# Attention stage of a three-stage kernel: the outputs of a unit in front of the transposes of unit u-2, the first expert matrix loaded two units later, its high parts made in units 8 and 9

## What is computed

```python
# attention: q, k, v are (4, 8, 576, 64)
kv = np.einsum('bhsd,bhse->bhde', k, v)
out = np.einsum('bhsd,bhde->bhse', q, kv)
rms = np.sqrt(np.mean(out * out, axis=-1, keepdims=True) + 1e-06)
x = out / rms * g_norm                       # then heads side by side: x is (2304, 512)
# dense mixture, 4 experts, w1 (512, 1024), w2 (1024, 512)
for e in range(E):
    out += p[:, e:e + 1] * (np.maximum(x @ w1[e], 0.0) @ w2[e])
# then a routed mixture: one of 8 experts for each row
```

## Time and profile before

| | us |
|---|---|
| median of 3 runs | 1134.98 |
| lowest and highest run | 1133.81, 1137.16 |
| the profiled execution, its time | 1131.23 |
| span of that execution (first to last instruction) | 1129.6 |

### The profile page before, as it was taken

One profiled execution on the slowest core, in us unless ns is written; L12 is line 12 of the kernel. 1 busy time (PEld: TensorE's weight loads), 2 busy tenths in 40 slices (PEclk: granted clock), 3 DMA queues, 4 the chain that ended last, 5 costly groups with the idle time before them and its releaser, 6 DMA issues.

```text
span 1129.6 us, 18534 instructions
## 1 busy us (share of the span) xinstructions
PE 1110.4 (98%) x6144; PEld 972.7 (86%) x6145; DVE 728.1 (64%) x1183; ACT 456.2 (40%) x814; POOL 653.3 (58%) x608
## 2 busy tenths in 40 slices
PE   8999999999999999999999999999999999999997
PEld 8888899988998898988998898889977888888885
DVE  4877887888775878888875878888753222222221
ACT  4773454444634444444534444444332222222221
POOL 2586877799868777799868777778331111111101
PEclk9999999999999999999999999999999999999999
DMA  9955778777712358777812258777398259479970
GB/s 242 264 153 185 269 267 288 281 251 273 262 38 75 109 167 304 276 258 271 273 41 75 93 179 303 254 272 266 134 376 315 84 202 393 138 307 383 344 279 15
DMA packets 103073, 252.97 MB, mean 224 GB/s; under 512 B 8318, under 2 KB 48254, under 8 KB 94811
## 3 DMA queue, kind: packets, MB, share of 16 engines
q1 hardware_dynamic: 98080, 237.54, 60.8%
q0 software_dynamic: 4720, 14.46, 3.5%
q10 hardware_dynamic: 203, 0.05, 0.0%
HBM read 173.09 MB, written 79.98 MB: 224 GB/s over the span
## 4 chain that ended last, share of the span: by engine, by line
PE 92%; DVE 3%; ACT 2%; DMA 1%; issue 1%; POOL 0%; SPq 0%; POOLq 0%; DVEq 0%; ACTq 0%
PE ps L1403 29%; PE ps L1405 28%; PE ps L1404 28%; PE ps L1591 2%; PE ps L1361 1%; PE ps L1568 1%; DMA q<-in_q_dram 1%; PE ps L1483 1%; PE ps L1331 1%; DMA row_tile<-dispatched_rows 1%; PE ps L1508 1%; DVE x_rows L1034 0%; DVE attn_rows L955 0%; PE ps L1372 0%; PE ps L1344 0%
## 5 line engine op out<-in xcount | busy, mean ns | idle before, releaser
L1403 PE MATMUL ps<-x_ops_hi,w_hi 128*128 128x384 f32 x672 | 226.4, 337 | 1.9 <-DVE sum L1004 1.9
L1403 PE MATMUL ps<-w_hi,hT_hi 128*128 128x512 f32 x576 | 226.8, 394 | 0.0
L1405 PE MATMUL ps<-x_ops_hi,w_lo 128*128 128x384 f32 x672 | 225.7, 336 | 0.0
L1405 PE MATMUL ps<-w_hi,hT_lo 128*128 128x512 f32 x576 | 225.2, 391 | 0.0
L1404 PE MATMUL ps<-x_ops_lo,w_hi 128*128 128x384 f32 x672 | 225.2, 335 | 0.0
L1404 PE MATMUL ps<-w_lo,hT_hi 128*128 128x512 f32 x576 | 225.0, 391 | 0.0
L1034 DVE SCALAR_TENSOR_TENSOR x_rows<-ps,dense_probs,x_rows 128x512 f32<-128x512 f32 x270 | 189.8, 738 | 15.6 <-PE ps L1405 15.3
L534 POOL TENSOR_TENSOR w_lo<-w_raw,w_hi 128x512 fp32r<-128x512 f32 x96 | 147.8, 1560 | 12.3 <-ACT w_hi L749 8.0
L652 POOL DMA_INDIRECT out_dram<-y_rows,row_ids x22 | 22.1, 1002 | 226.2 <-DVE y_rows L1280 122.8
L1155 DVE TENSOR_TENSOR rhT_lo<-ps,rhT_hi 128x512 fp32r<-128x512 f32 x44 | 28.5, 686 | 166.3 <-ACT rhT_hi L870 166.2
L1403 PEld LDWEIGHTS ps<-x_ops_hi,w_hi 128*128 128x128 f32 x672 | 126.1, 188 | 6.5 <-DVE sum L1004 3.2
(11 more groups left out here) (224 smaller groups left out, 1973.1 us busy)
## 6 DMA issues: line engine op xcount, KB each, us to landing
w_slots<-split_parts SPq DMA_DIRECT2D x64, 1024.0 KB, 6.1
w_raw<-in_moe_w_dram SPq DMA_DIRECT2D x96, 512.0 KB, 3.6
ahead_raw<-in_moe_w_dram SPq DMA_DIRECT2D x64, 512.0 KB, 6.7
split_parts<-ahead_hi SPq DMA_DIRECT2D x64, 512.0 KB, 4.1
split_parts<-ahead_lo SPq DMA_DIRECT2D x64, 512.0 KB, 5.7
row_tile<-dispatched_rows POOLq DMA_DIRECT2D x19, 257.0 KB, 5.8
kv<-in_k_dram SPq DMA_DIRECT2D x16, 288.0 KB, 8.0
kv<-in_v_dram SPq DMA_DIRECT2D x16, 288.0 KB, 8.3
```

Of the source, the lines that this page charges most:

```text
L1403: mm(out_, ah, bh, start=(first and m == 0), stop=False, skip_group_check=not final or not first)
L1405: last = mm(out_, al, bh, start=False, stop=(final and m == n - 1), skip_group_check=not final or not first)
```

## The change

There are four edits. On PE, outputs(u) now stands ahead of transposed(u-2); since it then writes a PSUM bank that unit u-2 used, it waits for o_scaled of that unit. The fillers ahead of unit 0 go from 12 to 8. On SP the load of the first w1 moves from the loads of unit 4 to those of unit 6. On ACT square(u) stands ahead of write_x(u-2), and w1_highs(0) of round 6 is cut in two: the raw highs in round 8, the sum highs in round 9. POOL and DVE keep their order. Line numbers behind the edits grow by 2 and then by 4.

```diff
                 load_unit(u, u % KVS)
-                if u == KVS:
+                if u == KVS + 2:
                     load_w1(0)
...
                 if u >= 1:
                     root(u - 1)
+                square(u, u % 2)
                 if u - 2 >= X_ON_ACT:
                     write_x(u - 2)
-                square(u, u % 2)
                 for i, at_ in zip(X_ORDER, (5, 7, 10, 11, 11, 12, 12)):
                     if u == at_:
                         x_high(0, i)
-                if u == 6:
-                    w1_highs(0)
+                if u == 8:
+                    w1_raw_highs(0)
+                if u == 9:
+                    w1_sum_highs(0)
                 if u == UNITS - 2:
                     w1_raw_highs(1)
             w1_sum_highs(1)
...
             def outputs(u, s):
 
+                if u >= 2:
+                    pe.wait_ge(o_scaled, u - 1)
                 pe.wait_ge(in_copied, 3 * u + 3)
...
-            fillers(WARM)
+            fillers(2 * WARM // 3)
             products_in(0, 0, 32)
...
+                outputs(u, u % 2)
                 if u >= 2:
                     transposed(u - 2, u % 2)
-                outputs(u, u % 2)
```

## The result

The changed kernel took 1136.77 us (median of 20 runs, 1134.16 to 1140.26), the kernel before 1134.29 us (median of 20 runs, 1130.49 to 1137.9). The ratio is 1.0027, with a 95% interval of 1.0018 to 1.0036: about 2.5 us by the medians, 3.1 by the ratio. It is slower by a little less than the 0.3% that the prediction named as its bound. Forecast were +2.5 us and, as the likeliest verdict, a difference too small to be told from none.

What follows compares the result with a forecast made beforehand. POOL's fixed list was taken as the new bound: x sums 3.9 us later cancel the attention's gain and put product 3 at 75.9, 2.5 us later. So 1134.98 + 2.5 = 1137.5 us, range 1132.5 to 1140.5.

Steps and rivals of the forecast that it cites:

- The chain behind the x sums: POOL to ACT to PE: from first x sum 16.4 us to last x low, 19.2 to second w1's sums; then 3.2 to product 3.
- The slack of 1.4 us: At the hand-over: POOL's sums of the second w1 end at 68.8, ACT reads them at 70.22.
- The fillers: Start of PE: 12 to 8 saves 1.0 to 1.55 us there, lost at the next transfer wait; worth 0 at the end.
- Rival B: POOL's lateness falls into ACT's slack and the attention's gain stays: 2.4 us faster, 1132.6 us; chance 0.15.
- Rival C: ACT's waits are shorter than worked out; loss and gain cancel within 1 us of zero, 1135 us; chance 0.13.
- the time of the x sums: POOL's first x sum starts at 53.5 against 49.59, 3.9 us later, 6.1 behind the sum highs of round 9.
- the floor of the transfers: Attention stage: transfers at 262 GB/s, 3.4 us a unit; v of unit 10 lands at 42.4, PE cannot start before.
- the wait at unit 5: PE at 25.69: w1's 2.0 us load no longer stands ahead, so the wait goes; PE up to 2 us earlier there.
- The bound that I had put on the x sums: Latest first x sum on POOL: 55.9, 6.3 us later than before, if PE wins nothing by round 9.
- The stall of round 11: ACT's x_high waits for POOL's x sums until 57.2; unit 14 starts at 59.6, so the 2 us won are gone.
- Rival D: DVE sets the pace and rounds win nothing by round 9: +4.9 us plus 0.5 in rounds 14 and 15, 1140 to 1141; chance 0.12.

Runs made afterwards that it cites:

- after: The changed kernel with all four edits, against the kernel before: 1136.77 us, ratio 1.0027.
- order_only: Kernel before with only the new orders on PE (outputs ahead of transposes) and ACT (square ahead of write of x): 1131.97 us, ratio 0.9983.
- after_fill: Changed kernel plus eight filler matmuls in front of unit 7's wait for its v; against the kernel before: 1137.03 us, ratio 1.0030.
- pool_late: Kernel before with four extra POOL subtractions, 7.1 us in all, ahead of the x sums: 1133.92 us, ratio 1.0019.
- xhighs_13_14: Changed kernel with ACT's four x highs that wait for x sums moved to rounds 13 and 14; against the kernel before: 1138.2 us, ratio 1.0053.
- highs_7_8: Changed kernel with first w1 loaded at unit 4, raw highs in round 7, sum highs in round 8; against the kernel before: 1133.05 us, ratio 1.0001.
- lows_first: Changed kernel with POOL's first two x lows ahead of the first w1's lows; against the kernel before: 1133.42 us, ratio 0.9992.
- lows_first_78: Changed kernel with POOL's first two x lows ahead of w1's lows and w1 highs in rounds 7 and 8; against the kernel before: 1130.44 us, ratio 0.9973.
- late_highs: Kernel before with only the first w1's move: load at unit 6, highs in rounds 8 and 9: 1137.49 us, ratio 1.0032.
- fill8_only: Kernel before with eight fillers in front of unit 0 instead of 12, nothing else: 1131.91 us, ratio 0.9998.
- early_highs: Changed kernel with first w1 loaded at unit 4, raw highs in round 6, sum highs in round 7; against the kernel before: 1131.31 us, ratio 0.9983.
- order_fill8: Kernel before with the new orders on PE and ACT and eight fillers, w1 load and highs unmoved: 1131.24 us, ratio 0.9974.

## Why the prediction was right, and where it was not

**What held.** *The chain behind the x sums,* in every length. From the first x sum to the end of the last x low I had 16.4 us; it is 56.49 to 72.84, 16.35. To the end of the second w1's sums 19.2; it is 19.25. From the sum highs to product 3 3.2; it is 3.02. From copy_in(13) to unit 14 1.59; it is 1.58. *The slack of 1.4 us* at the sum highs of the second w1: in the eight kernels in which ACT waits there for POOL's sums (after, order_only, after_fill, pool_late, xhighs_13_14, highs_7_8, lows_first, lows_first_78), product 3 starts 22.30 to 22.35 us behind the first x sum, where the kernel before had 23.82; the slack was 1.5. In late_highs it is 22.79, by the stall of round 11, and in the four others, where ACT does not wait for POOL at that place, 23.06 to 23.80. *The fillers* are worth nothing (fill8_only). *Rival B* fell: it needed an x sum by about 51. Reordering POOL's list alone, from the change to lows_first, gave 3.5 per mille, with POOL at 57% of the span and PE at 98%. The rule beside rival B, the Trainium skill's (Perfetto Trace Analysis, Identifying the Most-Contended Engine), to improve the engine of the highest occupancy first, taken by itself passes over POOL; these runs speak against it. *Rival C* fell with the interval of 1.0018 to 1.0036.

**The term that was mis-sized** is the time of the x sums. I wrote 53.5, from sum highs done at 47.4; they were done at 50.39, and the x sum started at 56.49, 6.1 behind them as worked out. All 3.0 us were lost ahead of outputs(9), which I had near 44 and which started at 47.08. Two things made them:
First, the floor of the transfers, which I took from one execution and called one rate. The v of unit 10 landed at 44.2 in this profile instead of 42.4: 1.8 us. Across the fourteen profiles these same transfers, seen from 9 to 60 us, ran at 246 to 272 GB/s.
Second, PE was not at that floor. The w1 load moved from in front of unit 5 to in front of unit 7, and so did the wait, which grew from 0.41 + 0.40 to 1.92 + 0.43 us. I wrote that the wait at unit 5 goes; it did, and came back two units later. Behind it the clock fell to 0.52 and the outputs took 2.77 for 1.48. From unit 8 on PE had rounds of 3.30 us without a wait between them, and reached unit 10 at 45.68, 1.5 us after its data. (Of the 3.3 us of both together I had allowed for 0.25.) I had priced only what a wait takes, not the slow stretch that follows it.
The bound that I had put on the x sums, 55.9 with nothing won by round 9, was itself passed by 0.6 us: outputs(9) were 0.6 us later than before. That they could be later I had not allowed.

**The stall of round 11** is there by its mechanism, with its size off by the same 3.0 us: unit 14 at 62.56 for 59.6. Unit 15 is off by 4.1, at 67.45 for 63.4, with the slow stretch between them. What it adds, 3.43 us of an idle PE and then a window at clock 0.50, I had not counted either; at product 3 it is covered by POOL's lateness, as xhighs_13_14 shows with 78.29 for 78.80.

**Rival D** put its point of decision at outputs(9) less than 0.8 us earlier, and this execution is beyond it; its +4.9 at product 3 is nearer to the 5.4 measured there than the forecast's 2.5. Its mechanism isn't the one at work, though: from 39 to 42, at full clock, DVE does not set the pace, with 1.94 of 3 us against 3.00 of PE. Nor did the runs reach its 1140.

**Why +2.5 came out all the same.** By the profiled execution the term should have cost 5.4 us at product 3, and the runs have 2.5 to 3.1. The table shows a difference between the last two columns that goes with the order of PE: with the transposes first (late_highs, pool_late, fill8_only) the runs and product 3 agree within 0.7 us; with the outputs first the runs are 1.4 to 3.2 us better than product 3 says, in all but xhighs_13_14. So with the outputs first the timed runs have something that the profiled executions don't show at product 3. It isn't in the stages behind either: from product 3 to the end of the span the profiled executions take 1056.2 to 1056.9 us with the transposes first and 1056.7 to 1059.4 with the outputs first. The mean transfer rate of the profiles goes with it (263 to 272 GB/s against 246 to 262), but with one profile each that is a correlation and no more. So the agreement of the number is luck. The working led to product 3 at 75.9, and the execution that it can be held against has 78.80. Something that the working left out gives back about as much in the timed runs: either a gain of the outputs first, or an x sum that is less late in most runs than in the profiled one. No trace of a second execution tells which. The sign, and POOL's list as its cause, were right on their own account.

## What to carry to other kernels

An engine that is idle for 84% of a stretch can still decide the end, if its list has a fixed order and something early in it is pushed back: add up its list from the pushed-back item to whatever the bound engine waits for, and subtract the slack at that reader (here 1.5 us). Before a producer is moved later, ask what stands behind its consumer in the list of every engine; moving two unrelated instructions, 3.6 us of work, ahead of the wait took the kernel from 1.0027 to 0.9992, and one round less of delay on top to 0.9973. And price an idle gap of the matmul engine with what comes behind it as well, and a floor from transfers with the rates of several executions.

## What the runs showed of the hardware

*The clock behind a gap.* Gaps of 3.43 us (the change), 3.49 (late_highs) and 4.72 (xhighs_13_14) were each followed by a window of 3 us with a granted clock of 0.50, and so was the one of 1.92 + 0.43 at unit 7 of the change, with 0.52. Shorter gaps went either way, and not by their length. Behind the wait of 0.96 + 0.38 us at unit 5 of highs_7_8 the outputs took 2.77 us for 1.48:

```profile
26.40 0.92 PE L1346 MATMUL ps<-kv 96*64 96x64 f32 x24 [0.96 <-DMA kv<-in_v_dram]
27.70 0.83 PE L1353 MATMUL ps<-ident,q 96*128 96x96 f32 x6 [0.38 <-DMA q<-in_q_dram]
28.32 2.77 PE L1365 MATMUL ps<-kv_blocks,qT 128*96 128x128 f32 x12
```

Behind gaps of 1.59 (early_highs), 1.66 (order_fill8) and 1.91 + 0.37 us (lows_first) they took 1.48. Two windows of lows_first:

```profile
33.00:36.00 3.00, 1.82 (x34) 1.72 (x35) 1.33 (x2) 0.16 (x2) 2.92 (x4) 1.00 1.14 256
36.00:39.00 3.00, 2.95 (x47) 2.69 (x46) 2.06 (x5) 1.93 (x5) 0.35 (x1) 1.00 1.13 257
```

The Trainium skill (TensorE: Matmul & The Clock Gate, What's actually happening) has it that idleness brings the throttle back. The longer gaps agree. What decides at 1 to 2 us the runs here don't show. Nor do they show where the waits come from that a trace calls issue: up to 1.28 us in after_fill, 1.24 in early_highs and 1.12 in pool_late, and 0.33 in the change.

*The first matmuls.* The first group of fillers ran at half pace in the changed kernel too. Its timeline:

```profile
2.21 3.78 PE L1333 MATMUL ps<-ident 128*128 128x128 f32 x16 [2.21 <-POOL eps L486]
5.92 1.55 PE L1346 MATMUL ps<-kv 96*64 96x64 f32 x24
...
10.21 0.92 PE L1346 MATMUL ps<-kv 96*64 96x64 f32 x24
```

16 records take 3.78 us (0.24 each, where the earlier trace rows has 0.19 and 0.12), and the first unit's group 1.55 where the next takes 0.92. The windows of the profile give a granted clock of 1.00 from 2 to 6 us, so the slow pace of the start does not show in that figure. The bound that I had for fewer fillers (a slow stretch that goes on for longer) is thus real, and hidden by the first waits for transfers, as fill8_only shows with 0.9998.

*The transfers.* At the same DMA share of 1.13 to 1.14 the rate from 9 to 60 us was between 246 GB/s (the change, highs_7_8) and 272 (late_highs). Whether the order of PE has a part in it, or only the execution, is open.
